# Coarse scores a slot earlier, window loads ahead of raw loads, and column sums by two rounded products with ones

## The reference

```
# 1. attention, summed from a coarse and a local part
q_d, k_d, v_d = means over groups of 4 positions           # 144 of 576
out_d   = softmax(q_d k_d^T / 8) v_d                       # repeated 4 times
out_loc = softmax(q k^T / 8 where |i-j| < 4) v
x = (out_up + out_loc) as [4, 576, 512]
# 2. block with normalization
mu, var = mean(x), mean((x-mu)^2)                          # over the 512 columns
x = x + relu(((x-mu)/sqrt(var+1e-6) * g) @ w_ch1) @ w_ch2  # 512 -> 2048 -> 512
# 3. block with shifted mixing
xk = mu_k*x + (1-mu_k)*x_prev ; xr likewise
out = sigmoid(xr @ w_r) * (relu(xk @ w_k)^2 @ w_v)         # 512 -> 1024 -> 512
```

## Time and profile before

| | us |
|---|---|
| median of 3 runs | 782.68 |
| profiled execution | 782.57 |
| its span in the profile | 780.7 |
| TensorE busy (97%) | 755.7 |
| DVE busy (55%) | 433.0 |
| ACT busy (35%) | 269.5 |
| POOL busy (29%) | 225.2 |

### The profile page before, as it was taken

One profiled execution on the slowest core, in us unless ns is written; L12 is line 12 of the kernel. 1 busy time (PEld: TensorE's weight loads), 2 busy tenths in 40 slices (PEclk: granted clock), 3 DMA queues, 4 the chain that ended last, 5 costly groups with the idle time before them and its releaser, 6 DMA issues.

```text
span 780.7 us, 15717 instructions
## 1 busy us (share of the span) xinstructions
PE 755.7 (97%) x6412; PEld 693.8 (89%) x6412; DVE 433.0 (55%) x797; ACT 269.5 (35%) x640; POOL 225.2 (29%) x260
## 2 busy tenths in 40 slices
PE   5799999999999999999999999999999999999997
PEld 5589999999999999989999999998888888888886
DVE  5967654434654344553443433466687576766655
ACT  5655422223123223223222321455433434423322
POOL 5266654133343224434312313003111111111101
PEclk9999999999999999999999999999999999999999
DMA  9982441220441022252011001731103002010010
GB/s 193 235 271 45 95 90 29 51 64 7 81 94 39 13 55 55 46 96 57 10 29 39 2 14 34 274 109 35 51 1 108 1 9 72 1 55 1 0 55 28
DMA packets 117959, 49.67 MB, mean 64 GB/s; under 512 B 96640, under 2 KB 106880, under 8 KB 117888
## 3 DMA queue, kind: packets, MB, share of 16 engines
q1 hardware_dynamic: 117888, 48.68, 24.9%
HBM read 39.20 MB, written 9.45 MB: 62 GB/s over the span
## 4 chain that ended last, share of the span: by engine, by line
PE 90%; SPq 3%; ACT 2%; issue 2%; DVE 2%; DMA 1%; POOL 0%; POOLq 0%; DVEq 0%; ACTq 0%
PE psH L955 26%; PE psY L972 23%; PE psH L1006 12%; PE psY L1025 12%; PE psA L988 6%; SPq L533 2%; PE psA L872 2%; PE psA L903 2%; PE psA L820 1%; ACT prob L1099 1%; PE psA L848 1%; PE psA L833 1%; PE psA L883 1%; DMA v_win<-in_v_dram 1%; DMA k_first<-in_k_dram 0%
## 5 line engine op out<-in xcount | busy, mean ns | idle before, releaser
L1565 DVE SCALAR_TENSOR_TENSOR h_lo<-psH,h_hi 128x288 fp32r<-128x288 f32 x128 | 58.4, 456 | 202.3 <-ACT h_hi L1273 202.3
L972 PE MATMUL psY<-h_hi,w_hi 128*128 128x288 f32 x512 | 158.5, 310 | 0.1
L955 PE MATMUL psH<-xc_hi,w_hi 128*128 128x288 f32 x512 | 156.1, 305 | 2.4 <-DVE xc_lo L1437 2.4
L955 PE MATMUL psH<-xc_lo,w_hi 128*128 128x288 f32 x512 | 152.2, 297 | 0.0
L955 PE MATMUL psH<-xc_hi,w_lo 128*128 128x288 f32 x512 | 151.8, 297 | 0.0
L972 PE MATMUL psY<-h_hi,w_lo 128*128 128x288 f32 x512 | 150.9, 295 | 0.0
L972 PE MATMUL psY<-h_lo,w_hi 128*128 128x288 f32 x512 | 150.9, 295 | 0.0
L1273 ACT ACTIVATE h_hi<-psH 128x288 fp32r<-128x288 f32 x128 | 52.5, 410 | 258.2 <-PE psH L955 258.1
L794 POOL TENSOR_TENSOR relu_k<-relu_k 128x512 f32<-128x512 f32 (+1 forms) x40 | 39.0, 975 | 246.9 <-ACT relu_k L1236 246.9
L955 PEld LDWEIGHTS psH<-xc_hi,w_hi 128*128 128x128 f32 x512 | 97.1, 190 | 5.5 <-issue 4.6
L972 PEld LDWEIGHTS psY<-h_hi,w_hi 128*128 128x128 f32 x512 | 96.1, 188 | 3.7 <-issue 1.3
(11 more groups left out here) (169 smaller groups left out, 1333.4 us busy)
## 6 DMA issues: line engine op xcount, KB each, us to landing
w_raw<-in_moe_w_ch_dram SPq DMA_DIRECT2D x8, 1024.0 KB, 7.4
v_win<-in_v_dram SPq DMA_DIRECT2D x84, 56.0 KB
x_scratch<-x SPq DMA_DIRECT2D x8, 576.0 KB, 4.0
out_dram<-gate SPq DMA_DIRECT2D x18, 256.0 KB, 2.2
raw<-in_q_dram SPq DMA_DIRECT2D x112, 36.0 KB, 2.1
raw<-in_k_dram SPq DMA_DIRECT2D x96, 36.0 KB, 1.9
v_raw<-in_v_dram SPq DMA_DIRECT2D x12, 288.0 KB
x_sh<-x_scratch SPq DMA_DIRECT2D x3, 1026.0 KB, 5.5
```

Source lines behind the costliest of these rows:

```text
L955: ins = mm(psH[:, m % 2, 0:N], ws[a][:, kt, f * P:(f + 1) * P], xx[bb][:, kt], start=(kt == 0 and i == 0), stop=(kt == KT - 1 and i == 2))
L972: ins = mm(psY[:, d, 0:N], ws[a][:, f, d * P:(d + 1) * P], hs[bb][:, m % 2], start=(f == 0 and i == 0), stop=(f == NF1 - 1 and i == 2))
L1565: nc.vector.scalar_tensor_tensor(out=h_lo[:, m % 2], in0=psH[:, m % 2, 0:N], scalar=0.0, in1=h_hi[:, m % 2].bitcast(F32), op0=ALU.max, op1 ...
```

## The change

Three edits and what they need. (1) Sd part 1 moves from slot 5 to slot 4. (2) SP issues the value windows of a slot ahead of its raw loads. (3) For units 1 to 7 the M and V products are no longer one float32 product of `ones` and `xs[:, 0]`: ACT copies the sum, rounded, to `sum_hi`, DVE subtracts it from the sum into `sum_lo`, and TensorE multiplies rounded ones with both. The two steps of M stand two slots behind AV 1 (slot 23), those of V four slots behind M (slot 28). `sum_hi` lies in the memory of `diag`; `sum_lo` is new, so what is placed behind it moves by 1152 bytes per partition, and a filler aligns `kh_hi`. Unit 0 keeps the old form.

```diff
-    LATER = [(2, "Sd", 0), (5, "Sd", 1),
+    LATER = [(2, "Sd", 0), (4, "Sd", 1),
...
-                ("AV", 0): [("x_out", 0, 0)], ("AV", 1): [("x_out", 1, 0), ("x_out", 2, 0)],
-                ("M", 0): [("centre", 0, 0), ("lo_x", 0, 1)], ("V", 0): [("var", 0, 0)]}
+                ("AV", 0): [("x_out", 0, 0)], ("AV", 1): [("x_out", 1, 0), ("x_out", 2, 0), ("x_lo", 0, 2)],
+                ("M", 0): [("centre", 0, 0), ("lo_x", 0, 1), ("sq_lo", 0, 4)], ("V", 0): [("var", 0, 0)]}
...
-                ("M", 0): [("hi_x", 0, 0), ("square", 0, 1)]}
+                ("AV", 1): [("x_hi", 0, 2)],
+                ("M", 0): [("hi_x", 0, 0), ("square", 0, 1), ("sq_hi", 0, 4)]}
...
-        diag = sb(ctx, "diag", [P, NW_U, W])
+        L = ExitStack()
+        diag = sb(L, "diag", [P, NW_U, W])
+        L.close()
+        sum_hi = sb(ctx, "sum_hi", [P, N], F32R)
+        sum_lo = sb(ctx, "sum_lo", [P, N], F32R)
...
+        sb(L, "before_kh", [P, (LINE - nc.sbuf_base % (2 * LINE)) % (2 * LINE) // 4])
...
+        ones_r = sb(ctx, "ones_r", [P, P], F32R)
...
                 if slot in V_LOAD:
                     load_v_sum(*V_LOAD[slot])
-                for x_ in flips_at(slot):
-                    if HALF <= flip_of[x_] < len(flips) - RAW:
-                        load_later(flip_of[x_] + RAW)
                 for kind, u, n in steps_at(slot):
                     for part in parts_of(kind, u, n):
                         if kind == "AV" and NW_U * u + part + 2 < NWIN:
                             load_window(NW_U * u + part + 2)
+                for x_ in flips_at(slot):
+                    if HALF <= flip_of[x_] < len(flips) - RAW:
+                        load_later(flip_of[x_] + RAW)
...
+            nc.gpsimd.memset(ones_r[:].bitcast(F32), 1.0).then_inc(consts, 1)
...
-                if u >= 1 and n == 0:
-                    pool.wait_ge(var_done, u)
+                if u == 1 and n == 0:
+                    pool.wait_ge(var_done, 1)
+                elif u >= 2 and n == 0:
+                    pool.wait_ge(sum_lo_made, 2 * (u - 1))
...
+            def ones_by_sums(dst):
+                mm(dst, ones_r[:], sum_hi[:], start=True, stop=False)
+                return mm(dst, ones_r[:], sum_lo[:], start=False, stop=True)
...
             def mean(u):
...
+                    pe.wait_ge(sum_lo_made, 2 * u - 1)
+                    ones_by_sums(dst).then_inc(mean_done, 1)
...
             def variance(u):
...
+                    pe.wait_ge(sum_lo_made, 2 * u)
+                    ones_by_sums(dst).then_inc(var_done, 1)
...
+            def hi_sum(u, i):
+                if i == 0:
+                    act.wait_ge(x_summed, NW_U * (u + 1))
+                    act.wait_ge(var_made, u)
+                else:
+                    act.wait_ge(sq_summed, u + 1)
+                    act.wait_ge(mean_done, u + 1)
+                copy(sum_hi[:], xs[:, 0]).then_inc(sum_hi_made, 1)
...
+            def lo_sum(u, i):
+                dve.wait_ge(sum_hi_made, 2 * (u - 1) + i + 1)
+                if i == 0:
+                    dve.wait_ge(var_done, u)
+                else:
+                    dve.wait_ge(mean_done, u + 1)
+                nc.vector.tensor_tensor(sum_lo[:], xs[:, 0], sum_hi[:].bitcast(F32), ALU.subtract).then_inc(sum_lo_made, 1)
```

More of the change, by code:

```diff
@@ L326, in fused_kernel @@
         sq_summed = sem("sq_summed")
+        sum_hi_made = sem("sum_hi_made")
+        sum_lo_made = sem("sum_lo_made")
         mean_done = sem("mean_done")
@@ L905, in values @@
                 ins.then_inc(av_done, 1)
+            def ones_by_sums(dst):
+                mm(dst, ones_r[:], sum_hi[:], start=True, stop=False)
+                return mm(dst, ones_r[:], sum_lo[:], start=False, stop=True)
             def mean(u):
                 i = place_of["M", u, 0]
-                pe.wait_ge(x_summed, NW_U * (u + 1))
                 wait_bank_out(pe, i)
-                mm(pairs[pair_at(i)][:, 0, 0:N], ones[:], xs[:, 0], start=True, stop=True).then_inc(mean_done, 1)
+                dst = pairs[pair_at(i)][:, 0, 0:N]
+                if u == 0:
+                    pe.wait_ge(x_summed, NW_U)
+                    mm(dst, ones[:], xs[:, 0], start=True, stop=True).then_inc(mean_done, 1)
+                else:
+                    pe.wait_ge(sum_lo_made, 2 * u - 1)
+                    ones_by_sums(dst).then_inc(mean_done, 1)
             def variance(u):
                 i = place_of["V", u, 0]
-                pe.wait_ge(sq_summed, u + 1)
                 wait_bank_out(pe, i)
-                mm(pairs[pair_at(i)][:, 0, 0:N], ones[:], xs[:, 0], start=True, stop=True).then_inc(var_done, 1)
+                dst = pairs[pair_at(i)][:, 0, 0:N]
+                if u == 0:
+                    pe.wait_ge(sq_summed, 1)
+                    mm(dst, ones[:], xs[:, 0], start=True, stop=True).then_inc(var_done, 1)
+                else:
+                    pe.wait_ge(sum_lo_made, 2 * u)
+                    ones_by_sums(dst).then_inc(var_done, 1)
             def attend(slot):
@@ L1051, in _ @@
             values(0, 2)
-            pe.wait_ge(consts, 6)
+            pe.wait_ge(consts, 7)
             mean(0)
@@ L1191, in attend @@
                         od_o(u, n)
+                    elif what in ("x_hi", "sq_hi"):
+                        hi_sum(u, int(what == "sq_hi"))
                     elif what == "hi_x":
@@ L1486, in attend @@
                         x_o(u, n)
+                    elif what in ("x_lo", "sq_lo"):
+                        lo_sum(u, int(what == "sq_lo"))
                     elif what == "centre":
```

## The result

The changed kernel takes 775.6 us (median of 4 runs, 775.12 to 776.24) against 783.8 (four runs of the kernel before, 781.73 to 785.26; three of them gave the 782.68 from which the forecast started): ratio 0.9898, interval 0.987 to 0.9925, so 1.0% faster. The forecast was 777.0, and 775.6 lies at the lower edge of its own range (775.6 to 778.6). The profiled execution took 776.24 with a span of 774.4; the span fell by 6.3 us (forecast: 5.5).

What follows compares the result with a forecast made beforehand. TensorE, busy 755.7 of 780.7 us, was taken as the bound, so only its queue or waits count. Gains of 9.5 us less 4.0 given back leave 5.5 off 782.57: 777.1, forecast 777.0, range 775.6 to 778.6.

Steps and rivals of the forecast that it cites:

- Ones products: TensorE's M and V products of units 1 to 7: two rounded products save 0.22 us each, at most 3.1 us.
- the low half: DVE's subtraction ahead of M ends barely in time: M late by 0.05 us in five passes, 0.25 us.
- V of unit 1: DVE's subtraction stands behind a transpose waiting for its DMA and a group sum, so V waits 1.24 us.
- PdT: Turned coarse probabilities on TensorE: seven waits for ACT's exponentials go with the earlier scores, gaining 4.2 us.
- Sd 1: Coarse scores at slot 4 wait for the bank: 0.45 us each in passes 2 to 6, 0.26 in pass 1.
- Pass 7: The L972 group waits for the fourth y_tmp, whose chain hangs on POOL, so V's 0.22 us is lost.
- Loads: Value windows ahead of raw loads on SP: values product's two waits in passes 2 and 4 go, gaining 2.5 us.
- Sum: Gains of 9.5 us less 4.0 given back: net 5.5 us against the profiled run.
- 1: Rival, 17%: no new waits; ACT's read of Sd 0 and pass 0's load come in time, 773.2 us.
- 2: Rival, 20%: the low part is late in every unit, each M by 0.5 us, 780.4 us.
- 3: Rival, 8%: the 1152-byte shift puts moving tiles on worse addresses and stretches products; 789.4 us at 8 ns each.
- 4: Rival, 7%: the order of the loads gains nothing, as windows are held by another wait (av_done); 779.6 us.

Runs made afterwards that it cites:

- the kernel without it: On the changed kernel, DVE subtracts for V ahead of the transposes and group sums of its slot: 775.85 us, ratio 0.9903.
- the second profile: The changed kernel run once more, unaltered, on the same chip as its parts: 776.16 us, ratio 0.9903 to the kernel before.

## Why the prediction was right, step by step

- **Ones products:** 0.22 for each, as worked out (13.24 to 13.02), and the low half was never late in front of M. The 0.25 us put down for it is too much; the unseen subtraction took 0.45 against the 0.46 taken and left 0.23, where the release of a product takes about 0.14. That POOL is idle beside the subtractions of passes 1 to 6 was wrong for V in passes 2 and 4; only slack hid it.
- **V of unit 1:** the mechanism is the one named, but its size is off. Against the 9.82 of the kernel without it, the wait was 1.06 (10.88; 1.13 in the second profile, 1.55 with the rounded products alone), not 1.24; the idle time in the rows is 0.90, 0.97 and 1.40. The size hangs on when the raw load lands. The prediction took its time from before. Counted from V of unit 0 the transpose behind it stood at 59.19 before and at 57.28, 57.36 and 59.52 in these three, while M1 came 1.72, 1.70 and 0 us earlier than before. Take 1.24, less what the load gained, plus what M1 gained: 1.05, 1.11 and 1.57.
- **PdT:** its waits are gone. The sum took them as 4.2 from the list of idle time. Pass 0 gave 1.72 where the list says 1.55, and in the others V's gain and the idle time less the new wait would make 0.21 us a pass where 0.33 was measured. So ending a wait of PdT gave 0.1 to 0.2 more than its idle time. That the rest is a pause at the restart is my reading, and no run tests it: ending the waits of Sd 1, 0.42 of idle time, shortened the passes by 0.41 to 0.44 and no more.
- **Sd 1:** five waits of 0.42 against 0.45 and one smaller in pass 1: L832 came at 110.79, about 0.2 after its place. The wait is 0.18 with the old V and 0.42 with the shorter one, so the chain is not moved by V, as said. It hangs on POOL's rstd; moving that removed the wait.
- **Pass 7:** V's gain is lost there (50.31 and 50.32).
- **Loads:** 1.00 and 1.69, together 2.7 for 2.5, again about 0.1 more each than the idle time (0.92 and 1.61).
- **Sum:** 7.09 from V of unit 0 on against 5.5. The 1.6 between is made of terms of one sign: PdT in pass 0 0.2, M1 to M2 0.3 (0.2 of it the wait of V), M 0.25, passes 2 to 6 0.6, loads 0.2. Five small terms were each sized on the careful side. None hid another, so the hit owes nothing to errors that cancel; but they add up, and bring the result to the edge of the forecast's own range.
- **Rivals:** 1 fell, there are new waits. 2 fell: M stands in step. 3 fell: L981's products have the same mean, 297 ns for both low products, as L955's. 4 fell: the loads alone give 2.7.

## What to carry to other kernels

When one engine is busy for 97%, list its waits, but follow each repaired one to the next user of the same buffer: moving the scores by a slot exchanged a wait of 0.44 us for one of 0.42. Ask of each new wait what the chain behind it hangs on, and whether something in it can wait itself (rstd could come 3.4 us later behind V at no cost in any distance; the additions could not). Work that is put into an in-order queue inherits every wait ahead of it, so look at the pass with the odd order, not only at the regular one. The same holds for a load that is moved: what stands behind its new place comes later.

## What the runs showed of the hardware

- A full-precision product of 128x288 delays what follows by 0.49 us, two rounded ones by 0.27.
- A DVE subtraction with two SBUF inputs of 288 columns takes 0.44 to 0.45 us alone and 0.84, 0.92 or 1.07 beside a POOL op that began before it; each time it ended 0.31 to 0.32 us after that op.
- A wait inside a group of products (L972 taking 2.32 us instead of 1.70) is missing from the list of the products' waits; the rows of their weight loads (0.24 and 0.34 us idle) and the distance to the next group show it.
